# A head's attention laid anew on its five steps, in a fused attention, gated convolution and spatial-gating kernel

## The chip, the cores and the metric

The kernel runs on one core of one Trainium2 chip. The time is the device time of one execution, in microseconds (us). Five engines work at once, each through its own queue of instructions in order: TensorE (PE, matmuls), VectorE (DVE), ScalarE (ACT), GpSimd (POOL) and SyncE (SP, which issues the DMAs). They wait for one another through semaphores.

## The reference

Three layers in a row, all in float32, for a batch of 4, 576 tokens, 8 heads of 64.

```
cum    = cumsum(max(s, 0))                          # per head
scores = q k^T / 8 + min(-(cum_i - cum_j), 0), causal mask
attn   = softmax(scores);  x = attn v               # 32 heads -> x (4, 576, 512)

gate = sigmoid(causal conv of 5 taps over x)        # depthwise
x    = (gate * (x w_val)) w_out

h    = relu(x w_in);  u, v = halves of h            # 512 each
v    = (v - mean) / sqrt(var + 1e-6)
v_s  = w_spatial v + b_spatial                      # over tokens
out  = (u * v_s) w_out2
```

## The kernel before

**Data.** Every product is made of float32r parts: a value is split into a high part (a ScalarE copy) and a low part (VectorE or GpSimd subtracts), and TensorE multiplies the parts. `w_out` and `w_in` are first multiplied together (`comb_mm`, 8 tiles of 4 products each, evicted by `comb_evict`), as nothing lies between them.

**Steps.** All work is written out along one list of steps, in `run`. At each step every engine's queue gets its part of what is called, in the order of the calls. Nothing synchronizes the steps; they only set the order in each queue. A head takes five steps (`NT` = 5 tiles of query rows, the last of 64 rows; tile i has 128(i+1) keys, the last 576); 32 heads make 160 steps. A batch's mixer (everything after attention) takes 40 steps and lies beside the attention of the next batch; the last one runs alone.

**A head.** For tile i: `scores` (TensorE) fills a bank of `score`; VectorE reduces it to the negated row maximum (L851); ScalarE's `exp` (L725) reads the bank and writes `prob`; `turn` transposes `prob` on TensorE (L1000) into one of two banks of `turned`, from which ScalarE copies the high part `pt_hi` (L734) and VectorE then subtracts the low part `pt_lo` (L869). There are two score banks: tiles 0 and 2 use one, 1 and 3 the other, and tile 4 lies over both, so `scores` of a tile waits for the exp of the tile before it in its bank. The products with v (`pv_...`, L1009) add up in `attn_o`; ScalarE copies the lower half (L744) and VectorE adds the upper (L877). Beside that, the sums of the exps are inverted on VectorE (`invert_sums`), transposed (`turn_sums`, L1031), copied (`keep_sums`), stored to DRAM and loaded again spread over partitions (`store_sums`, `spread_sums`), and GpSimd multiplies two heads' x by them (L659).

Before the change the steps of a head g are: tile 0 scored in its step 0, 1 in 1, 2 and 3 in 2, 4 in 4. Its tiles are turned in the steps of the next head: 0 and 1 in step 0, then one a step. The products with v come in steps 3 and 4 of the next head and step 0 of the one after, the combination there too. In a step, TensorE's mixer products come first, then scores, then turns; ScalarE copies the turned tile and then makes the exp.

**The mixer.** `mixer_schedule` gives each operation its step, counted from the batch's end of attention. `lead` is called first in a step and `tail` last. The units of products are "val" (8), "v" (5, each in two halves), "u" (8), "spatial" (8, of 15 matmuls each) and "out" (8). A tap is one of the five VectorE operations of a channel block's convolution (L894, L897); `tanh` makes the gate of it. `x_hi` and `x_lo` split x. "val" and "spatial" units are evicted by VectorE (L914, L918), the others by ScalarE; `stats`, `norm` and `split` normalize and split v.

**Weights.** `weights` gives piece n its high part in step 2 + n on ScalarE and its low part a step later, on GpSimd for even n and VectorE for odd; SyncE loads a piece seven ahead. `COMB_STEPS` lists the steps of the combined products. The late pieces (`w_spatial`, `w_out2`) come from `LATE_FROM` on.

Of the kernel before, what the change touches and what calls it, by code (L numbers as in the profile page):

```python
# [30 lines left out]
TAPS = 5  # L31
# [56 lines left out]


def build(nc, q, k, v, s, w_val, conv_w, w_out_t, w_in, w_spatial, b_spatial, w_out2, out_t):  # L90
# [8 lines left out]
    NH = B * H  # L99
# [33 lines left out]
    TURNED_IN = [(0, 1), (2,), (3,), (4,), ()]  # L133
    SLOTS = NC + 2
    EARLY = 3

    ctx = ExitStack()
    with ctx:
# [269 lines left out]
        def run(do):  # L408
# [15 lines left out]
            def weights(step):  # L424
                for n in range(FIRST_LOADS, len(PIECES)):
                    at = WEIGHTS_FROM + n if n < LATE_PIECE else LATE_FROM + n - LATE_PIECE
# [12 lines left out]
            def early(step):  # L439
                g, i = divmod(step, NT)  # L440
                if g < NH and i == EARLY:
                    call("scores", g, i)
                    call("exp", g, i)

            def attention(step):
                g, i = divmod(step, NT)
                if i == 0 and 0 <= g - 2 < NH:
                    call("pv_rest", g - 2)
                if i == 2 and 0 <= g - 1 < NH:
                    call("turn_sums", g - 1)  # L450
                    call("keep_sums", g - 1)
                if g < NH and i != EARLY:
                    call("scores", g, i)
                if 0 <= g - 1 < NH:
                    for n in TURNED_IN[i]:
                        call("turn", g - 1, n)
                    if i == 3:
                        call("pv_first", g - 1)
                    if i == 4:
                        call("pv_second", g - 1)  # L460
                if g < NH and i != EARLY:
                    call("exp", g, i)
                if i == 0 and 0 <= g - 1 < NH:
                    call("invert_sums", g - 1)
                if i == 0 and 0 <= g - 2 < NH:
                    call("combine", g - 2)
                if i == 0 and g + 1 < NH:
                    call("scale_q", g + 1)
                if i == (0 if g == 0 else 1) and g + 1 < NH:
                    call("split_qk", g + 1)  # L470
                    call("place_qk", g + 1)
                if step == 0:
                    call("more_weights")
                if i == 2 and g + 2 < NH:
                    call("load_qk", g + 2)
                if i == 3 and 0 <= g - 1 < NH:
                    call("store_sums", g - 1)
                if i == 3 and g < NH:
                    call("split_v", g)
                    if g + 1 < NH:  # L480
                        call("load_v", g + 1)
                if i == 4 and 0 <= g - 1 < NH:
                    call("spread_sums", g - 1)
# [131 lines left out]
        def _(pool):  # L615
# [38 lines left out]
            def combine(g):  # L654
# [24 lines left out]
            run({"setup": setup, "weights_lo": weights_lo, "split_qk": split_qk, "split_v": split_v, "combine": combine,  # L679
# [4 lines left out]
        def _(act):  # L684
# [51 lines left out]
            def combine(g):  # L736
# [27 lines left out]
            def evict(b, alone, unit):  # L764
# [4 lines left out]
                if kind == "v":  # L769
# [3 lines left out]
                    elif b > 0:  # L773
# [15 lines left out]
            def split(b, alone, unit):  # L789
# [4 lines left out]
                else:  # L794
# [5 lines left out]
                 "exp": exp, "turn": turn, "keep_sums": keep_sums, "combine": combine, "x_hi": x_hi, "tanh": tanh, "evict": evict, "split": split,  # L800
# [143 lines left out]
        def _(pe):  # L944
# [76 lines left out]
            def pv_second(g):  # L1021
                pe.wait_ge(pt_lo_done, NT * (g + 1))
                pv_part(g, (0, 1), False, NT - 1)

            def pv_rest(g):
# [95 lines left out]
            def mm(b, alone, unit, half):  # L1121
# [6 lines left out]
                if half == 1 or unit[0] != "v":  # L1128
                    ins.then_inc(unit_done, 1)

            run({"setup": setup, "scores": scores, "turn": turn, "pv_first": pv_first, "pv_second": pv_second,
                 "pv_rest": pv_rest, "turn_sums": turn_sums, "comb_mm": comb_mm, "mm": mm})
# [32 lines left out]
```

## Time and profile before

| | us |
|---|---|
| median of 3 runs | 579.08 (578.79 to 579.66) |
| profiled execution | 577.76 |
| its span, first to last instruction | 576.0 |
| TensorE busy | 519.5 (90%) |
| VectorE busy | 369.8 (64%) |
| ScalarE busy | 330.2 (57%) |
| GpSimd busy | 263.2 (46%) |
| mean granted TensorE clock | 0.97 of full |

Busy shares are averages over stretches with different limits: the first batch's attention, which has only weight work beside it, three batches of attention with a mixer beside it, and the last mixer alone. They have to be read stretch by stretch. `turn_sums` occurs once a head, always in the same step of it (step 7, 12, 17, ... before the change), so that its starts cut the trace into heads.

### The profile page before, as it was taken

To read this page: it belongs to the slowest core of one execution; us is meant where nothing else is said; L and a number is where in the kernel's file an instruction comes from. 1 tells how busy PE (TensorE), PEld (TensorE's weight loads), DVE (VectorE), ACT (ScalarE), POOL (GpSimd) and SP (SyncE) were. 2 spreads that over 40 slices of the span, in tenths; PEclk is the share of its full clock that TensorE was granted. 3 is DMA by queue.
4 is the path that set the end of the run, shared out by engine and by line. 5 is a ranking of instruction groups with operands and counts; after the bars stand their busy time and mean duration, and the time that the engine had idled before them with its cause. 6 is when DMAs were issued, how large, how long until landed. Compare 5 with 4: busy or idle time off the path is not lost. (4 is left out here: it accounts for less than half of the span.)

```text
span 576.0 us, 10408 instructions
## 1 busy us (share of the span) xinstructions
PE 519.5 (90%) x3472; PEld 452.9 (79%) x3472; DVE 369.8 (64%) x726; ACT 330.2 (57%) x844; POOL 263.2 (46%) x247
## 2 busy tenths in 40 slices
PE   1758787878898899999999999999999999999998
PEld 1446565656886699998887899998877999997997
DVE  7346677776865866666758675768677757565240
ACT  4457666665584755676566656666666655523322
POOL 5244544433487664633556745445558544003100
PEclk9968999986998999999999999999999999999999
DMA  6753444432253333244333222343333320200002
GB/s 182 200 157 100 127 131 119 105 84 63 60 151 83 84 84 79 69 109 119 85 87 103 71 71 52 101 136 95 83 84 84 84 63 13 73 20 2 1 2 82
DMA packets 46887, 50.34 MB, mean 87 GB/s; under 512 B 24881, under 2 KB 29137, under 8 KB 46834
## 3 DMA queue, kind: packets, MB, share of 16 engines
q1 hardware_dynamic: 46834, 49.68, 32.2%
q8 instruction: 28, 0.46, 0.3%
q14 instruction: 25, 0.20, 0.1%
HBM read 25.83 MB, written 4.95 MB: 53 GB/s over the span
## 5 line engine op out<-in xcount | busy, mean ns | idle before, releaser
L725 ACT ACTIVATE prob<-score,neg_max 128x128 f32<-128x128 f32 (+4 forms) x159 | 90.2, 567 | 114.0 <-DVE neg_max L851 113.7
L869 DVE TENSOR_TENSOR pt_lo<-turned,pt_hi 128x128 fp32r<-128x128 f32 (+4 forms) x160 | 77.7, 489 | 69.7 <-ACT pt_hi L734 69.2
L851 DVE TENSOR_REDUCE neg_max<-score 128x1 f32<-128x128 f32 (+4 forms) x159 | 84.7, 533 | 40.0 <-PE score L981 35.1
L638 POOL TENSOR_TENSOR q<-raw,raw_hi 64x576 fp32r<-64x576 f32 x32 | 46.5, 1453 | 105.6 <-issue 60.7
L734 ACT ACTIVATE pt_hi<-turned 128x128 fp32r<-128x128 f32 (+4 forms) x160 | 66.8, 434 | 40.5 <-PE turned L1000 39.1
L979 PE MATMUL score<-k,q 68*128 68x256 f32 (+2 forms) x128 | 52.7, 412 | 30.8 <-ACT prob L725 17.2
L1000 PE MATMUL turned<-ident,prob 128*128 128x128 f32 (+1 forms) x480 | 71.1, 269 | 0.0
L1009 PE MATMUL attn_o<-pt_hi,v_hl 128*128 128x256 f32 (+2 forms) x224 | 66.9, 316 | 1.6 <-DVE pt_lo L869 1.6
L897 DVE SCALAR_TENSOR_TENSOR u_t<-x_t,taps,u_t 128x576 f32<-128x576 f32 x64 | 61.3, 957 | 0.7
L1041 PE MATMUL mix<-ws_hl,act_a 128*128 128x288 f32 (+1 forms) x405 | 59.2, 298 | 0.0
L1009 PE MATMUL attn_o<-pt_lo,v_hl 128*128 128x256 f32 (+2 forms) x224 | 59.1, 298 | 0.0
L406 POOL TENSOR_TENSOR act_b<-u_t,act_b 128x288 fp32r<-128x288 f32 x48 | 41.1, 861 | 37.9 <-ACT act_b L797 37.6
L979 PEld LDWEIGHTS score<-k,q 68*128 68x128 f32 x128 | 25.9, 202 | 38.4 <-issue 20.9
L659 POOL TENSOR_TENSOR x_t<-x_t,r_bc 128x576 f32<-128x576 f32 x16 | 25.7, 1605 | 66.2 <-DVE x_t L877 56.6
L1041 PEld LDWEIGHTS mix<-ws_hl,act_a 128*128 128x128 f32 (+1 forms) x405 | 55.0, 188 | 0.0
L1000 PEld LDWEIGHTS turned<-ident,prob 128*128 128x128 f32 (+1 forms) x480 | 48.3, 146 | 8.0 <-issue 6.0
L1041 PE MATMUL mix<-wc_hl,act_b 128*128 128x512 f32 (+1 forms) x204 | 54.4, 405 | 0.0
L1041 PE MATMUL mix<-act_b,wc_hl 128*128 128x288 f32 x312 | 46.2, 299 | 4.1 <-ACT work L776 4.1
L1041 PE MATMUL mix<-act_a,wv_hl 128*128 128x288 f32 x312 | 47.7, 303 | 1.0 <-DVE wc_hl L902 1.0
L1041 PE MATMUL mix<-act_b,w_hl 128*128 128x288 f32 x324 | 48.2, 298 | 0.0
L1009 PEld LDWEIGHTS attn_o<-pt_hi,v_hl 128*128 128x128 f32 x224 | 43.2, 193 | 6.0 <-DVE pt_lo L869 2.1
L651 POOL TENSOR_TENSOR v_hl<-v_raw,v_hl 128x320 fp32r<-128x320 f32 x32 | 37.0, 1155 | 23.8 <-ACT v_hl L716 23.6
(149 smaller groups left out, 1055.1 us busy)
## 6 DMA issues: line engine op xcount, KB each, us to landing
q<-raw_hi SPq DMA_DIRECT2D x64, 144.0 KB
k<-raw_hi SPq DMA_DIRECT2D x64, 144.0 KB
raw<-in_q SPq DMA_DIRECT2D x32, 144.0 KB, 2.8
raw<-in_k SPq DMA_DIRECT2D x32, 144.0 KB, 2.9
r_bc<-r_dram SPq DMA_DIRECT2D x32, 144.0 KB, 2.9
out<-work SPq DMA_DIRECT2D x32, 144.0 KB, 1.8
v_raw<-in_v SPq DMA_DIRECT2D x32, 128.0 KB, 2.1
u_t<-in_moe_w_in SPq DMA_DIRECT2D x7, 256.0 KB, 4.4
```

Source lines behind the costliest of these rows:

```text
L406: eng.tensor_tensor(lo, src, hi.bitcast(F32), ALU.subtract).then_inc(lo_done, 1)
L638: pool.tensor_tensor(q2[p][0:D, :], raw[0:D, :], raw_hi[0:D, :].bitcast(F32), ALU.subtract).then_inc(lo_made, 1)
L651: pool.tensor_tensor(v_hl[p][:, :, D:2 * D], v_raw[:, :, :], v_hl[p][:, :, 0:D].bitcast(F32), ALU.subtract).then_inc(v_lo_done, 1)
L725: act.activation(prob_view(i), score_view(g, i), ACT.Exp, bias=neg_max[p][0:rows[i], i:i + 1], accum_out=row_sum[p][0:rows[i], i:i + 1]).t ...
L734: act.activation(pt_view(pt_hi, i), turned_view((g + i) % 2, i), ACT.Copy).then_inc(pt_hi_done, 1)
L851: dve.tensor_reduce(neg_max[g % 2][0:rows[i], i:i + 1], score_view(g, i), AX_X, ALU.max, negate=True).then_inc(max_done, 1)
L869: dve.tensor_tensor(pt_view(pt_lo, i), turned_view((g + i) % 2, i), pt_view(pt_hi, i).bitcast(F32), ALU.subtract).then_inc(pt_lo_done, 1)
L897: dve.scalar_tensor_tensor(out=to, in0=src, scalar=w, in1=to, op0=ALU.mult, op1=ALU.add).then_inc(conv_step, 1)
L979: pe.matmul(score[:, base:base + n], q1[p][0:D + 4, qs], k1[p][0:D + 4, 0:n], start=True, stop=False)
L1000: ins = pe.transpose(turned[:, (g + i) % 2, j * rows[i]:(j + 1) * rows[i]], prob[0:rows[i], at:at + P], ident[0:rows[i], 0:rows[i]])
L1009: ins = pe.matmul(attn_o[:, O_OFF + lo:O_OFF + hi], v_hl[g % 2][:, j, :], t[:, at:at + hi - lo], start=(j == 0 and t is pt_hi), stop=(j == ...
L1041: ins = pe.matmul(o, a(ha), b(hb), start=(n == 0 and t == 0), stop=(n == len(pairs) - 1 and t == 2))
```

## The change

The five steps of a head are laid out anew (`scoring`, `turning`, `joining`, `moving` in place of `early` and `attention`):

- tiles 0 and 1 are scored in step 0, 2 in step 1, 3 in step 2, 4 in step 3, none in step 4;
- tiles are turned in the same head: 0 and 1 in step 2, 2 in step 3, 3 in step 4, and 4 in step 0 of the next head;
- `pv_first` stands in step 4, the rest of the products with v in step 1 of the next head (one call `pv` in place of `pv_second` and `pv_rest`), the combination in step 2, the multiplication by the inverted sums (now called `divide`) in step 3;
- in every step scores and exp come first on all engines, then turns, then the mixer's leading part; so ScalarE makes the exp before it copies a turned tile;
- splitting and placing q and k goes from step 1 of the head before to step 4, two heads before; loads and DMAs of the sums go with the new steps;
- the mixer starts two steps earlier, its taps, statistics, norms and splits get other steps, the combined products and late weight pieces too;
- `turn_sums` no longer waits for the combination; `pv_first` does.

```diff
-    for c, step in enumerate((1, 3, 4, 6)):
-        put(lead, step, "x_hi", c)
+    for c, step in enumerate((-1, 1, 2, 5)):
+        put(tail, step, "x_hi", c)
         put(tail, step, "x_lo", c)
-    for n, step in enumerate((-17, -16, -16, -14, -12, -11, -11, -9, -7, -6, -2, -2, -1, 1, 3) if first else
-                             (-22, -21, -21, -17, -16, -12, -11, -11, -9, -7, -2, -2, -1, 1, 3)):
-        put(tail, step, "tap", n // TAPS, n % TAPS)
-    for t, step in enumerate((7, 8, 8, 9, 9)):
+    for n in range(3 * TAPS):
+        put(tail, (-21 if first and n < TAPS else -16) + n, "tap", n // TAPS, n % TAPS)
+    for t, step in enumerate((5, 5, 6, 6, 7)):
         put(tail, step, "tap", 3, t)
-    for c, step in enumerate((-5, -4, 5, 10)):
+    for c, step in enumerate((-10, -5, 0, 8)):
         put(lead, step, "tanh", c)
-    step = 8
+    step = 6
...
-        put(tail, (18, 21, 22, 24, 26)[j], "stats", j)
-        put(tail, (21, 23, 24, 26, 28)[j], "norm", j)
-        put(tail, (23, 24, 25, 28, 29)[j], "split", ("v", j, 0))
+        put(tail, step + 2, "stats", j)
+        put(tail, step + 4, "norm", j)
+        put(tail, step + 5, "split", ("v", j, 0))
...
-    TURNED_IN = [(0, 1), (2,), (3,), (4,), ()]
+    SCORED_IN = [(0, 1), (2,), (3,), (4,), ()]
+    TURNED_IN = [(), (), (0, 1), (2,), (3,)]
...
-        COMB_STEPS = [6, 7, 9, 11] + [n for n in range(12, H * NT + 8) if n % NT != 0 and n != 17]
+        COMB_STEPS = [7, 9, 11, 12] + [n for n in range(13, H * NT + 6) if n % NT != 0 or n in (H * NT, H * NT + 5)]
-        LATE_FROM = H * NT + 8
+        LATE_FROM = H * NT + 7
+        LATE_STEPS = [LATE_FROM + n for n in (0, 1, 3, 5, 6, 8, 10, 11, 13)]
...
+            def scoring(step):
+                g, i = divmod(step, NT)
+                if g < NH:
+                    for n in SCORED_IN[i]:
+                        call("scores", g, n)
+                        call("exp", g, n)
+            def turning(step):
+                g, i = divmod(step, NT)
+                if i == 0 and 0 <= g - 1 < NH:
+                    call("turn_sums", g - 1)
+                    call("turn", g - 1, NT - 1)
+                    call("keep_sums", g - 1)
+                if g < NH:
+                    for n in TURNED_IN[i]:
+                        call("turn", g, n)
+            def joining(step):
+                g, i = divmod(step, NT)
+                f = g - 1
+                if i == 1 and 0 <= f < NH:
+                    call("pv", f)
+                    call("copy_low", f)
+                if i == 2 and 0 <= f < NH:
+                    call("combine", f)
+                if i == 3 and 0 <= f < NH:
+                    call("divide", f)
+                if i == 4 and g < NH:
+                    call("pv_first", g)
+                    call("invert_sums", g)
+            def moving(step):
+                g, i = divmod(step, NT)
+                f = g - 1
+                if step == 0:
+                    call("scale_q", 1)
+                    call("split_qk", 1)
+                    call("place_qk", 1)
+                    call("more_weights")
+                if step == 1:
+                    call("split_v", 0)
+                if i == 1 and 0 <= f < NH:
+                    call("store_sums", f)
+                if i == 1 and g + 2 < NH:
+                    call("load_qk", g + 2)
+                if i == 2 and g + 1 < NH:
+                    call("load_v", g + 1)
+                if i == 2 and 0 <= f < NH:
+                    call("spread_sums", f)
+                if i == 4 and g + 1 < NH:
+                    call("split_v", g + 1)
+                if i == 4 and g + 2 < NH:
+                    call("scale_q", g + 2)
+                    call("split_qk", g + 2)
+                    call("place_qk", g + 2)
...
+                scoring(step)
+                turning(step)
                 mixer(0, step)
                 comb(step)
-                attention(step)
-                early(step + 1)
+                joining(step)
+                moving(step)
                 weights(step)
-                if step == 7:
+                if step == 5:
                     call("bias_rows")
                 mixer(1, step)
...
-                pe.wait_ge(r_copied, g + 1)
+                wait(pe, r_copied, g)
+                wait(pe, o_added, g)
                 pe.wait_ge(pt_lo_done, NT * g + 2)
...
             def turn_sums(g):
                 pe.wait_ge(inv_done, g + 1)
-                wait(pe, o_added, g)
```

## Rows read from the trace of the kernel before

**Rows 1.** page, part 1: busy us of each engine, share of the span, instructions
```profile
PE 519.5 (90%) x3472; PEld 452.9 (79%) x3472; DVE 369.8 (64%) x726; ACT 330.2 (57%) x844; POOL 263.2 (46%) x247
```

**Rows 2.** windows: length, busy us (count) per engine, TensorE clock, DMA share, GB/s
```profile
24.37:46.85 22.48, 12.54 (x58) 9.22 (x56) 9.43 (x21) 10.64 (x26) 7.05 (x5) 0.75 0.46 121
...
46.85:137.26 90.41, 73.25 (x412) 54.70 (x411) 65.09 (x127) 58.50 (x151) 41.20 (x29) 0.92 0.42 109
...
46.85:142.64 95.79, 76.99 (x429) 57.51 (x427) 68.49 (x133) 62.73 (x161) 44.11 (x31) 0.91 0.41 107
...
221.53:342.28 120.75, 118.51 (x846) 105.68 (x844) 84.86 (x168) 76.53 (x202) 65.23 (x62) 1.00 0.34 90
...
326.14:342.28 16.14, 16.14 (x124) 15.09 (x122) 11.96 (x22) 10.37 (x28) 7.29 (x8) 1.00 0.30 75
...
373.39:387.55 14.16, 14.16 (x110) 13.12 (x108) 9.71 (x18) 9.44 (x24) 6.01 (x4) 1.00 0.49 138
```

**Rows 3.** timeline of PE: start us, us, engine, line, operation [idle before <- releaser]
```profile
35.50 0.76 PE L1041 MATMUL mix<-act_b,ws_hl 128*128 128x512 f32 x1 [4.16 <-DVE act_b L370]
...
44.29 0.47 PE L1041 MATMUL mix<-act_b,ws_hl 128*128 128x512 f32 x1 [3.35 <-DVE act_b L370]
...
142.64 1.65 PE L1041 MATMUL mix<-act_a,wv_hl 128*128 128x288 f32 x6
```

**Rows 4.** waits: us in total, times, longest us
```profile
PE score L979 <- ACT prob L725: 17.2, 19, 2.4
...
PE score L988 <- ACT prob L725: 6.0, 6, 1.7
...
PE mix L1041 <- DVE act_b L370: 7.5, 2, 4.2
...
DVE pt_lo L869 <- ACT pt_hi L734: 69.2, 99, 2.2
```

**Rows 5.** ScalarE's groups by form: count, busy us, mean ns, idle before
```profile
L725 ACT ACTIVATION_READ_ACCUMULATOR prob<-score,neg_max 128x1 f32 x128 | 25.5, 199 | 0.0
...
L725 ACT ACTIVATE prob<-score,neg_max 128x256 f32<-128x256 f32 x32 | 15.1, 471 | 15.3 <-DVE neg_max L851 15.1
...
L725 ACT ACTIVATE prob<-score,neg_max 128x512 f32<-128x512 f32 x32 | 22.0, 688 | 23.9 <-DVE neg_max L851 23.9
...
L725 ACT ACTIVATE prob<-score,neg_max 64x576 f32<-64x576 f32 x31 | 22.9, 737 | 67.2 <-DVE neg_max L851 67.2
...
L734 ACT ACTIVATE pt_hi<-turned 128x128 fp32r<-128x128 f32 x32 | 8.8, 275 | 25.1 <-PE turned L1000 25.1
...
L734 ACT ACTIVATE pt_hi<-turned 128x384 fp32r<-128x384 f32 x32 | 15.6, 488 | 8.8 <-PE turned L1000 8.5
...
L734 ACT ACTIVATE pt_hi<-turned 128x320 fp32r<-128x320 f32 x32 | 13.8, 431 | 1.4 <-PE turned L1000 1.4
```

**Rows 6.** page, part 5, VectorE's reduces and low parts, all forms together
```profile
L851 DVE TENSOR_REDUCE neg_max<-score 128x1 f32<-128x128 f32 (+4 forms) x159 | 84.7, 533 | 40.0 <-PE score L981 35.1
...
L869 DVE TENSOR_TENSOR pt_lo<-turned,pt_hi 128x128 fp32r<-128x128 f32 (+4 forms) x160 | 77.7, 489 | 69.7 <-ACT pt_hi L734 69.2
```

**Rows 7.** VectorE's groups by form
```profile
L897 DVE SCALAR_TENSOR_TENSOR u_t<-x_t,taps,u_t 128x576 f32<-128x576 f32 x64 | 61.3, 957 | 0.7
...
L877 DVE TENSOR_TENSOR x_t<-attn_o,x_t 64x576 f32<-64x576 f32 x32 | 24.0, 750 | 10.7 <-ACT x_t L744 10.6
...
L856 DVE TENSOR_SCALAR raw<-raw 64x576 f32<-64x576 f32 x32 | 15.1, 472 | 6.7 <-DMA raw<-in_k 6.2
...
L914 DVE SCALAR_TENSOR_TENSOR u_t<-u_t,mix 128x288 f32<-128x288 f32 x26 | 11.6, 444 | 5.6 <-PE mix L1041 5.6
```

**Rows 8.** line 897, the taps: duration ns min/median/max, first and last start
```profile
L897 DVE SCALAR_TENSOR_TENSOR u_t<-x_t,taps,u_t x64: 798/813/2025, 78.7 to 510.6; 128x576 f32<-128x576 f32 x64
```

**Rows 9.** timeline of VectorE, a tap and what follows it
```profile
101.26 0.81 DVE L897 SCALAR_TENSOR_TENSOR u_t<-x_t,taps,u_t 128x576 f32<-128x576 f32 x1
...
101.98 0.74 DVE L851 TENSOR_REDUCE neg_max<-score 64x1 f32<-64x576 f32 x1
```

More of the change, by code:

```diff
@@ L132, in build @@
     NS = len(SPLITS)
-    TURNED_IN = [(0, 1), (2,), (3,), (4,), ()]
+    SCORED_IN = [(0, 1), (2,), (3,), (4,), ()]
+    TURNED_IN = [(), (), (0, 1), (2,), (3,)]
     SLOTS = NC + 2
-    EARLY = 3
     ctx = ExitStack()
@@ L425, in weights @@
                 for n in range(FIRST_LOADS, len(PIECES)):
-                    at = WEIGHTS_FROM + n if n < LATE_PIECE else LATE_FROM + n - LATE_PIECE
+                    at = WEIGHTS_FROM + n if n < LATE_PIECE else LATE_STEPS[n - LATE_PIECE]
                     if step == at:
@@ L437, in comb @@
                         call("comb_evict", n)
-            def early(step):
+            def scoring(step):
                 g, i = divmod(step, NT)
[L441 to L445, printed above, removed]
+                if g < NH:
[3 more added lines that the diff above has]
+            def turning(step):
@@ L446, in attention @@
                 g, i = divmod(step, NT)
-                if i == 0 and 0 <= g - 2 < NH:
-                    call("pv_rest", g - 2)
-                if i == 2 and 0 <= g - 1 < NH:
+                if i == 0 and 0 <= g - 1 < NH:
                     call("turn_sums", g - 1)
+                    call("turn", g - 1, NT - 1)
                     call("keep_sums", g - 1)
-                if g < NH and i != EARLY:
-                    call("scores", g, i)
-                if 0 <= g - 1 < NH:
+                if g < NH:
@@ L455, in attention @@
                     for n in TURNED_IN[i]:
[L456 to L471, printed above, removed]
+                        call("turn", g, n)
[12 more added lines that the diff above has]
+                    call("invert_sums", g)
@@ L472, in attention @@
+            def moving(step):
+                g, i = divmod(step, NT)
+                f = g - 1
                 if step == 0:
+                    call("scale_q", 1)
+                    call("split_qk", 1)
+                    call("place_qk", 1)
                     call("more_weights")
-                if i == 2 and g + 2 < NH:
-                    call("load_qk", g + 2)
[L476 to L481, printed above, removed]
@@ L482, in attention @@
-                if i == 4 and 0 <= g - 1 < NH:
-                    call("spread_sums", g - 1)
+                if step == 1:
[3 more added lines that the diff above has]
+                if i == 1 and g + 2 < NH:
+                    call("load_qk", g + 2)
+                if i == 2 and g + 1 < NH:
+                    call("load_v", g + 1)
+                if i == 2 and 0 <= f < NH:
+                    call("spread_sums", f)
@@ L652, in split_v, with divide @@
                                    ALU.subtract).then_inc(v_lo_done, 1)
-            def combine(g):
+            def divide(g):
                 if g % 2 == 1:
@@ L677, in split @@
                     split_lo(pool, b, unit)
-            run({"setup": setup, "weights_lo": weights_lo, "split_qk": split_qk, "split_v": split_v, "combine": combine,
+            run({"setup": setup, "weights_lo": weights_lo, "split_qk": split_qk, "split_v": split_v, "divide": divide,
                  "stats": stats, "split": split})
@@ L734, in turn, with copy_low @@
                 act.activation(pt_view(pt_hi, i), turned_view((g + i) % 2, i), ACT.Copy).then_inc(pt_hi_done, 1)
-            def combine(g):
+            def copy_low(g):
                 a, h = divmod(g, H)
@@ L772, in evict @@
                         act.wait_ge(lo_done, NS * b + SPLIT[("val", n, 1)] + 1)
-                    elif b > 0:
+                    elif b == 0:
+                        wait_pieces(act, len(PIECES))
+                    else:
                         act.wait_ge(out_stored[2 * (n - NC + 1)], 16 * OUTS * b)
@@ L799, in _ @@
             run({"cumulate": cumulate, "bias_rows": bias_rows, "weights_hi": weights_hi, "split_qk": split_qk, "split_v": split_v,
-                 "exp": exp, "turn": turn, "keep_sums": keep_sums, "combine": combine, "x_hi": x_hi, "tanh": tanh, "evict": evict, "split": split,
+                 "exp": exp, "turn": turn, "keep_sums": keep_sums, "copy_low": copy_low, "x_hi": x_hi, "tanh": tanh, "evict": evict, "split": split,
                  "comb_evict": comb_evict})
@@ L1016, in pv_first, with pv @@
                 pe.wait_ge(v_lo_done, g + 1)
-                pe.wait_ge(r_copied, g + 1)
+                wait(pe, r_copied, g)
+                wait(pe, o_added, g)
                 pe.wait_ge(pt_lo_done, NT * g + 2)
                 pv_part(g, (0, 1), True, 1).then_inc(pv_first_done, 1)
-            def pv_second(g):
+            def pv(g):
                 pe.wait_ge(pt_lo_done, NT * (g + 1))
                 pv_part(g, (0, 1), False, NT - 1)
-            def pv_rest(g):
                 pv_part(g, (2, 3, 4), False, NT - 1).then_inc(pv_done, 1)
@@ L1129, in mm @@
                     ins.then_inc(unit_done, 1)
-            run({"setup": setup, "scores": scores, "turn": turn, "pv_first": pv_first, "pv_second": pv_second,
-                 "pv_rest": pv_rest, "turn_sums": turn_sums, "comb_mm": comb_mm, "mm": mm})
+            run({"setup": setup, "scores": scores, "turn": turn, "pv_first": pv_first, "pv": pv,
+                 "turn_sums": turn_sums, "comb_mm": comb_mm, "mm": mm})
 _INS = ["q", "k", "v", "s", "moe_w_val", "moe_conv_w", "moe_w_out", "moe2_w_in", "moe2_w_spatial",
```

## The prediction

> **What bounds the kernel now.** I read the shares of busy time first, then a table of stretches cut at the starts of `turn_sums`, then the waits, then single instructions. Over the span TensorE is busy 519.5 of 576.0 us [rows 1]. The stretches divide that [rows 2]. A whole overlapped batch, where attention and the mixer of the batch before run together, takes 120.75 us with TensorE busy 118.51 at full clock: TensorE sets the time there, and only 2.24 us a batch is idle. The first batch's attention is another regime. From 24.37 to 46.85 us TensorE is busy 12.54 of 22.48; over seven heads from 46.85 to 137.26 it is busy 73.25 of 90.41, VectorE 65.09. No engine is full there. The order in each queue sets the time. The waits say so [rows 4]: TensorE's scores wait for ScalarE's exp 17.2 + 6.0 us, and two combined-weight products wait 7.5 us for a weight's low part. Those two lie at 35.50 and 44.29 us [rows 3]. From where the mixer begins (142.64 us [rows 3]) the remaining work is TensorE's own, so the end is that work plus whatever TensorE loses; the change removes no matmul.
>
> **The change, part by part.** The sum is made for the profiled execution: 577.76 us, 1.8 more than its span. The median of the three runs is 1.3 above it; I move the median by the same difference.
>
> *(a) Combined-weight products on later steps.* They stood on steps 6, 7, 9, 11 and go to 7, 9, 11, 12; the pieces' own steps stay. The low part of piece 5 is made in step 8 and needed by the third product: one step later before, three after. Piece 7: made in step 10, needed in step 11 before, 12 after. The waits of 4.16 and 3.35 us [rows 3] hang on these two, and behind them in TensorE's queue stood a head's scores. They can go whole (-7.5), or come back as waits of the same scores for VectorE (0), because VectorE is busy only 9.43 of the 22.48 us but in long strings. I take -4.0. `bias_rows` moves from step 7 to 5 and may wait for its load there, beside a DMA wait that exists anyway: nothing.
>
> *(b) The mixer starts two steps earlier.* From step 12 to step 48 (46.85 to 142.64) is 35.6 steps in 95.79 us, 2.69 a step. Of that TensorE's attention work is small: a spatial head (15 matmuls a step) takes 16.14, one with 12 a step 14.16 [rows 2]; 15 matmuls more cost 1.98, 0.132 each, so 60 are 7.9 and a head's attention is 6.2, 1.25 a step. Two steps before the mixer less return 2 x (2.69 - 1.25) = -2.9. Between 0 (if the mixer then waits for its first input) and -2.9. In the new chain pv, combine, divide and x_hi lie on steps 1, 2, 3 and 5, x_lo on 5 and the product on 6; the DMA pair of the sums has steps 1 to 3. That fits, so I keep -2.9.
>
> *(c) Chain first: exp goes ahead of the turned tile's copy on ScalarE.* Before, ScalarE copied `pt_hi` and then made the exp, so VectorE's `pt_lo` followed its reduce nearly at once. After, in steps 0, 2 and 3 of a head VectorE's order is reduce, `pt_lo`, and `pt_lo` needs reduce, exp, `pt_hi` on ScalarE in turn. VectorE must be idle meanwhile, however much is queued behind (taps, evicts, combine). Durations from [rows 5], with 0.1 for the handovers: step 2: exp of tile 3 0.69 + read 0.10 beyond it + `pt_hi` 0.28 + 0.1 = 1.2, a little more for the second tile, 1.3; step 3: 0.74 + 0.10 + 0.49 + 0.1 = 1.4; step 0: exp 1 0.47 + 0.10 + `pt_hi` 0.43 + 0.1 = 1.1. That is 3.75 us of compulsory idle a head. Steps 1 and 4 have none. Before, the seven heads had 90.41 - 65.09 = 25.32 of VectorE idle, 3.62 each. So in the first batch the compulsory idle replaces an idle of the same size. Operations that follow one another start closer than they last (a tap at 101.26, the reduce at 101.98, for 0.81 [rows 9]), which takes perhaps 0.4 a head off; what is added is 0.5 for places where the queues still wait on each other. 3.84 against 3.62, times seven: +1.5. Bounds: -2.0 (no such places: 3.34) and +9 (each head also keeps the 1.2 or so by which the heads of before wait beyond one compulsory gap). What goes: tile 0's scores no longer stand one step behind tile 4's exp (tile 4 is now scored in step 3, step 4 scores nothing), which is most of the 23.2 us of score waits [rows 4]; late next is VectorE, not TensorE. `turn_sums` loses its wait for the combine; it is left waiting for `invert_sums`, queued on VectorE behind `pt_lo` 3. The wait for the combine passes to `pv_first`, two steps behind it, with the next head's scores queued after it: nothing.
>
> *(d) The same order in the overlapped batches.* Each has VectorE busy 84.86 of 120.75 [rows 2]; eight heads' compulsory idle add 30.0: 114.9, 95% of the time. On the mean it fits. It must also fit locally, as TensorE can only be led by about a step. A head costs VectorE five reduces 2.67, five `pt_lo` 2.44 [rows 6], combine 0.75 and scaling 0.47 [rows 7], 6.3, with the idle 10.1 (the two short ones of `invert_sums` I take as paid by the closer starts). A tap adds 0.72 (start to start [rows 9]), an evict of "val" or "spatial" 0.44 [rows 7]. Mixer steps 30 to 34 have five taps and five evicts now: 10.1 + 3.6 + 2.2 = 15.9 against TensorE's 16.14: just hidden. Steps 5 to 9 have the five taps of the last channel, one x_lo (as a combine, 0.75) and four evicts: 10.1 + 3.6 + 0.75 + 1.8 = 16.2 against 14.16: 2.0 not hidden. The other groups have 1 us or more to spare. Of the 2.24 idle before I leave half. So 2.0 + 1.1 - 2.24 = +0.9 a batch, and three such batches: +2.7. Bounds: -6.7 (all idle gone, the excess carried into the next head) and +15 (0.6 a head lost to coupling, near the 0.70 that one wait of `pt_lo` for `pt_hi` lasts: 69.2 over 99 [rows 4]).
>
> *(e) Moved and priced at nothing.* GpSimd's and SyncE's splits and placements of q and k go from step 1 of the head before to step 4 two heads before, so they have six steps instead of four; on SyncE they stand ahead of nothing but loads of two heads on. stats, norm and split of v come earlier, spread evenly; what consumes them keeps three steps. Late weight pieces are spread over 14 steps and are due at mixer step 30, as before. After the last attention TensorE is full before and after.
>
> The median tap lasts 0.81 and the mean 0.96, the longest 2.03 [rows 7, 8]; something blocks a few. The Trainium skill (SBUF — State Buffer, "SBUF: two separate sides") says that VectorE with two SBUF inputs and GpSimd share a port pair under an exclusive lock, so that the later of the two waits for the whole other instruction. That speaks against this change, since the splits of q and k now fall on step 4, and three taps of a batch fall there with them: by the rule VectorE would lose up to some 3 us a batch more, by the mean row 0.15 a tap, as today.
>
> Sum: -4.0 - 2.9 + 1.5 + 2.7 = -2.7. Profiled: 575.1; median: **576.4 us**.
>
> **The rivals.**
> *R1, slower: VectorE becomes the bound.* Place: `pt_lo` in steps 0, 2 and 3, waiting behind an exp that itself stands behind ScalarE's evicts and splits. If each of the three waits is 0.15 longer than its compulsory part, 0.45 a head over 31 heads is +14: 590.4. It decides early: from 0.13 a head (0.13 x 31 = 4) the kernel is slower than before. For it: the 95% of (d), and that VectorE already waits 69.2 us for `pt_hi` in the kind order. Against: TensorE's margin of about one step in most groups, and that the first batch's heads idle as much already. In the first batch the granted clock is 0.92 over the seven heads and 0.75 in the stretch before [rows 2], where TensorE idles most, and 1.00 in the overlapped batches. The Trainium skill (TensorE: Matmul & The Clock Gate, Part 1) says that an idle array falls to 1.2 GHz; so R1 would bring such stretches into the overlapped batches too, at a further price that no row here bounds.
>
> *R2, much faster: the queues never meet.* The weight waits go whole (-7.5), two steps -2.9, first batch -2.0, overlapped batches unchanged: -12.4, 566.7. For it: only 90.41 - 73.25 = 17 us of the seven heads is TensorE idle and nearly all of it waits for exp. Against: compulsory idle of VectorE stays.
>
> *R3, no change.* The ramp is bound by loads and by VectorE's own string, and the mixer's start is held by the sums' round trip through DRAM, so (a) and (b) bring nothing, while (c) and (d) cost nothing: 579.1. For it: 22.48 us for five steps, with DMAs in flight. Against: the step numbers of (a).
>
> **How the numbers follow.** Forecast 0.43, its own range 571 to 583; R1 0.25; R2 0.20; R3 0.12. About 0.2% (1.2 us) is what a measurement can tell from no change. Of the forecast's own case 0.6 lies under 577.9, 0.18 within the band, 0.22 above. Faster: 0.26 + 0.20 + 0.02 = 0.48; same: 0.08 + 0.07 = 0.15; slower: 0.09 + 0.25 + 0.03 = 0.37. The range takes in R2's value and most of R1's: 566 to 594.
>
> **What would show it.** (a): no TensorE wait for `act_b` low parts before the first head's combined tile is done, and `turn_sums` of head 1 before 43 us. (b): the first "val" product near 135 us. (c): `pt_lo` waits for `pt_hi` well above 69.2 us in total, near 32 x 3.75 = 120; score waits for exp far below 23; seven heads in 90 to 93 us. (d): overlapped batches of 120 to 122 us, with TensorE idle gathered in mixer steps 5 to 9. I am wrong if the overlapped batches grow by 3 us or more each or show a clock under 1.00 (R1), if the ramp keeps its 22 us (R3), or if batches fall under 119.

## The result, and the profile after

The changed kernel takes 628.81 us (628.38 to 630.34, 4 runs) against 578.93 of the kernel before on the same chip (578.61 to 579.66, 4 runs): 1.086 times as long (95% interval 1.084 to 1.089). 576.4 was forecast, with a range of 566 to 594.

Part 1 of the page, and the granted clock and busy slices of part 2, of the changed kernel:

```profile
PE 538.2 (86%) x3472; PEld 467.8 (75%) x3472; DVE 381.9 (61%) x726; ACT 323.0 (52%) x844; POOL 252.0 (40%) x247
...
PE   2586878767989889989799899978999999999998
...
PEclk9878888888789999999999999999999999999999
```

The matmuls are the same 3472. TensorE's busy time rose from 519.5 [rows 1] to 538.2 us, as more of them ran at the lower of its two clock levels (1.2 and 2.4 GHz): the mean granted clock fell from 0.97 to 0.945. The rest of the 50 us is idle. The windows are cut at the starts of the reciprocal in `invert_sums`, which occurs once a head. First come the first batch's heads 1 to 7 in the kernel before, cut in the same way, then the same heads and the second overlapped batch in the changed kernel.

```profile
41.94:118.71 76.77, 60.42 (x354) 44.60 (x355) 54.26 (x108) 50.34 (x131) 35.34 (x25) 0.97 0.43 115
```

```profile
42.29:136.94 94.65, 71.76 (x354) 55.63 (x354) 59.70 (x111) 49.38 (x131) 34.54 (x26) 0.82 0.36 97
292.75:427.40 134.65, 122.54 (x847) 107.74 (x845) 88.27 (x168) 74.50 (x202) 62.58 (x62) 0.99 0.31 81
```

Six heads of the first batch take 94.65 us where they took 76.77: 15.8 each against 12.8. TensorE's 354 matmuls in them last 71.76 us in place of 60.42, at a granted clock of 0.82 in place of 0.97, so part of the longer head is TensorE at its lower clock; no run took that part alone. VectorE's idle there is (94.65 - 59.70) / 6 = 5.8 us a head, against 3.75. An overlapped batch takes 134.65 where it took 120.75 [rows 2], with TensorE idle 12 us in it.

The waits of the whole kernel (us in total, times, longest):

```profile
DVE pt_lo L883 <- ACT pt_hi L746: 121.7, 105, 2.6
...
ACT raw_hi L723 <- DVE raw L870: 42.6, 24, 2.4
DVE neg_max L865 <- PE score L995: 31.5, 28, 4.2
PEld attn_o L1043 <- DVE row_inv L879: 30.8, 25, 2.1
PE attn_o L1043 <- DVE row_inv L879: 27.2, 23, 2.0
...
PE score L993 <- ACT prob L737: 22.4, 19, 7.2
...
PE score L1002 <- ACT prob L737: 13.7, 17, 2.0
```

L883, L746, L865, L1043, L723 and L870 are the lines 869, 734, 851, 1031, 711 and 856 of before. VectorE's wait for the high part went from 69.2 [rows 4] to 121.7, close to the 120 foretold. `turn_sums` (L1043) waited 2.4 us in all before, and for the combination; now it waits 27.2 for the inverse. The waits of scores for exp did not go; 23.2 became 36.1. ScalarE's wait to copy the scaled q (`raw_hi`) is new too; its row before was:

```profile
ACT raw_hi L711 <- DVE raw L856: 1.0, 2, 0.6
```

Before, VectorE scaled q in one step and ScalarE copied it in the next; now both are in step 4, with VectorE's part behind `invert_sums` and ScalarE's ahead of the next exp.

How these hang together shows in the chain of waits through one head of the first batch (start us, length, what the chain ran through; its pieces of "issue", time on no profiled work, are among those left out):

```profile
90.17 0.19 DVE row_inv L879
90.36 0.34 DVE raw L870
...
90.72 0.02 ACT raw_hi L723
...
91.31 0.15 ACT prob L737
...
91.81 0.69 PE score L993
...
92.95 1.39 PE mix L1053 x3
94.33 2.29 PE attn_o L1023 x10
96.63 0.59 PE score L993
...
97.74 0.70 DVE neg_max L865
...
99.05 0.19 ACT prob L737
99.24 0.44 ACT pt_hi L746 x2
...
100.20 0.69 DVE wc_hl L916
100.90 0.65 DVE x_t L891
101.55 0.68 DVE neg_max L865
...
103.08 0.38 ACT pt_hi L746
...
103.48 0.52 DVE pt_lo L883
...
104.57 0.75 DVE row_inv L877
```

The string runs: inverse, scaling of q, its copy on ScalarE, exp 0, scores 2, combined products, pv, scores 3, reduce 3, exp 3, copies, two other VectorE operations, reduce 4, exp 4, copy, low part, inverse. From one inverse to the next it passes through VectorE, ScalarE and TensorE in turn. (The view follows one chain back; it does not say how nearly another is as long.) VectorE's reduce at 97.74 had stood 4.20 us for scores that were queued behind pv, the rest of the products with v of the head before.

### The profile page after: what moved, and what is told of

Read it like the earlier page. It is cut to its first block, busy times and chain, and to the rows that moved or that the text cites. A ratio compares the mean times of both kernels' runs of the same rounds, so it can differ in the third digit from the quotient of the medians.

```text
span 626.6 us, 10373 instructions
## 1 busy us (share of the span) xinstructions
PE 538.2 (86%) x3472; PEld 467.8 (75%) x3472; DVE 381.9 (61%) x726; ACT 323.0 (52%) x844; POOL 252.0 (40%) x247
## 4 chain that ended last, share of the span: by engine, by line
PE 45%; DVE 27%; issue 11%; ACT 11%; DMA 3%; SPq 1%; POOL 1%; ACTq 0%; DVEq 0%; POOLq 0%
PE mix L1053 22%; PE attn_o L1023 7%; DVE neg_max L865 6%; DVE pt_lo L883 5%; PE attn_o L1053 4%; ACT pt_hi L746 4%; PE score L1053 3%; ACT prob L737 3%; DVE x_t L891 3%; DVE u_t L911 3%; PE score L993 3%; PE turned L1014 2%; PE score L994 2%; DVE act_a L895 2%; DVE row_inv L877 1%
## 5 line engine op out<-in xcount | busy, mean ns | idle before, releaser
L737 ACT ACTIVATE prob<-score,neg_max 128x128 f32<-128x128 f32 (+4 forms) x159 | 89.5, 564 | 157.6 <-DVE neg_max L865 157.1
L883 DVE TENSOR_TENSOR pt_lo<-turned,pt_hi 128x128 fp32r<-128x128 f32 (+4 forms) x160 | 77.6, 490 | 121.7 <-ACT pt_hi L746 121.7
L865 DVE TENSOR_REDUCE neg_max<-score 128x1 f32<-128x128 f32 (+4 forms) x159 | 82.3, 531 | 32.0 <-PE score L995 31.5
L993 PE MATMUL score<-k,q 68*128 68x256 f32 (+2 forms) x128 | 54.0, 422 | 34.5 <-ACT prob L737 22.4
L746 ACT ACTIVATE pt_hi<-turned 128x128 fp32r<-128x128 f32 (+4 forms) x160 | 64.0, 428 | 1.6 <-PE turned L1014 1.6
L1023 PE MATMUL attn_o<-pt_lo,v_hl 128*128 128x256 f32 (+2 forms) x224 | 64.6, 321 | 0.0
L911 DVE SCALAR_TENSOR_TENSOR u_t<-x_t,taps,u_t 128x576 f32<-128x576 f32 x64 | 64.3, 1004 | 0.4
L663 POOL TENSOR_TENSOR v_hl<-v_raw,v_hl 128x320 fp32r<-128x320 f32 x32 | 32.1, 1002 | 68.8 <-ACT v_hl L728 68.7
L1014 PEld LDWEIGHTS turned<-ident,prob 128*128 128x128 f32 (+1 forms) x480 | 50.2, 146 | 8.0 <-issue 1.9
L1053 PE MATMUL mix<-act_a,wv_hl 128*128 128x288 f32 x312 | 51.9, 319 | 3.4 <-DVE act_a L895 2.8
L1023 PEld LDWEIGHTS attn_o<-pt_hi,v_hl 128*128 128x128 f32 x224 | 48.7, 217 | 1.8 <-DVE pt_lo L883 0.4
L1023 PEld LDWEIGHTS attn_o<-pt_lo,v_hl 128*128 128x128 f32 x224 | 48.7, 217 | 1.6
```

The costliest lines, as they stand in the source:

```text
L663: pool.tensor_tensor(v_hl[p][:, :, D:2 * D], v_raw[:, :, :], v_hl[p][:, :, 0:D].bitcast(F32), ALU.subtract).then_inc(v_lo_done, 1)
L737: act.activation(prob_view(i), score_view(g, i), ACT.Exp, bias=neg_max[p][0:rows[i], i:i + 1], accum_out=row_sum[p][0:rows[i], i:i + 1]).t ...
L746: act.activation(pt_view(pt_hi, i), turned_view((g + i) % 2, i), ACT.Copy).then_inc(pt_hi_done, 1)
L865: dve.tensor_reduce(neg_max[g % 2][0:rows[i], i:i + 1], score_view(g, i), AX_X, ALU.max, negate=True).then_inc(max_done, 1)
L883: dve.tensor_tensor(pt_view(pt_lo, i), turned_view((g + i) % 2, i), pt_view(pt_hi, i).bitcast(F32), ALU.subtract).then_inc(pt_lo_done, 1)
L911: dve.scalar_tensor_tensor(out=to, in0=src, scalar=w, in1=to, op0=ALU.mult, op1=ALU.add).then_inc(conv_step, 1)
```

## The experiments

Each ratio is to the kernel before, measured together with the run (578.4 to 578.8 us). The changed kernel is 628.8.

**1. The sums turned at the end of step 0.**

```diff
                 if i == 0 and 0 <= g - 1 < NH:          # turning
-                    call("turn_sums", g - 1)
                     call("turn", g - 1, NT - 1)
-                    call("keep_sums", g - 1)
...
+                if i == 0 and 0 <= f < NH:              # joining
+                    call("turn_sums", f)
+                    call("keep_sums", f)
```

> One edit to the changed kernel: turn_sums and keep_sums are called at the end of a head's step 0 (behind the mixer's unit and the combined product) instead of ahead of the turn of tile 4. Theory T (TensorE's queue stands behind the inverted sums: 27.2 us of waits of L1043 for L879, with the turn of tile 4, the next product and the next scores queued behind it, and VectorE then idle for those scores): most of the 27 us and part of what follows comes back, 595 to 607 us, and those waits fall under 8 us. Theory C (VectorE's compulsory idle, exp ahead of the copy of the turned tile): the wait only moves, 624 to 630. Theory M (the mixer's new steps): 622 to 630.

619.5 us (1.071, 1.060 to 1.081). The waits of TensorE for the inverse fell from 27.2 to 7.0, but only 9 us came back. Part of that wait was slack that the next one took: the scores' wait for exp in the row of 22.4 grew to 39.4.

**2. The turned tile copied ahead of the exp.**

```diff
                 scoring(step)        # now scores alone
                 turning(step)
+                raising(step)        # exp of SCORED_IN
```

> One edit to the changed kernel: in each step ScalarE copies the turned tiles first and makes the exps after, as before the change; steps of a head stay. Theory C: VectorE's waits for pt_hi fall from 121.7 us to 70 or less, and since VectorE sets the pace in the first batch and about half of the overlapped ones, 590 to 603 us. Theory T: exp 4 is made later, so the sums are inverted no earlier, 620 to 632. Theory M: 620 to 630.

603.6 us (1.044, 1.036 to 1.051): 25.2 us of the 50 hang on this order alone. (`exp` is taken out of `scoring` and called in `raising`.) The waits of `pt_lo` fell from 121.7 to:

```profile
DVE pt_lo L889 <- ACT pt_hi L752: 42.2, 54, 2.0
```

Heads 1 to 7 gained little by it. There these waits fell from 21.5 us to 4.9, but VectorE's waits for scores rose from 12.6 to 20.9, and the window shrank only from 94.65 to:

```profile
41.88:134.36 92.48, 70.00 (x354) 54.48 (x354) 60.92 (x110) 50.73 (x131) 35.17 (x26) 0.83 0.37 99
```

**3. Mixer first in a step, as before the change.**

```diff
+                mixer(0, step)
+                comb(step)
                 scoring(step)
                 turning(step)
-                mixer(0, step)
-                comb(step)
```

> One edit to the changed kernel: in each step the mixer's leading part and the combined product are called ahead of scores, exps and turns again, on every engine. Under theory T and C alike this adds a unit of TensorE work between the inverse and turn_sums, and puts pv directly ahead of a product instead of ahead of tile 3's scores: T says 605 to 618 (the wait is covered by the unit, 1.6 to 2 us of it in the overlapped batches, nothing in the first batch beyond 0.7); C says 622 to 632 (ScalarE's order within the chain is the same); a theory that chain-first order itself is what costs says under 595.

641.1 us (1.108, 1.100 to 1.116). Slower than any of the three theories had it. Chain-first between engines' queues is not what costs; in this layout it is worth 12 us.

**4. The schedule of before for mixer, combined products and late pieces,** under the changed attention (`mixer_schedule`, `COMB_STEPS`, `LATE_FROM` restored).

> The changed kernel's attention with the schedule of before for the mixer, the combined products and the late weight pieces (the mixer starts at step 48 again). Theory M (taps, x_lo and statistics on wrong steps fill VectorE): under 605. Theories T and C: the loss is in the attention's own chain, 625 to 636, with a first batch as slow per head (15.4 to 15.8 us) as in the changed kernel.

634.7 us (1.097, 1.090 to 1.105). So the loss is in the attention, and that group of edits returns 6 us there.

**5. Edits 1 and 2 together.**

> The two edits of the first two runs together: turned tiles copied ahead of the exps, turn_sums and keep_sums at the end of step 0. If the two losses are separate (25.2 and 9.3 us of the changed kernel's 628.8), 594 to 597. If the wait for the sums was only a wait that the late pt_lo caused, nothing beyond the first edit: 602 to 605. If the chain of a head in the first batch is bound elsewhere (pv ahead of tile 3's scores), its heads stay at 14.5 to 15 us in both cases.

594.5 us (1.029, 1.021 to 1.036): 34.3 us back against 25.2 + 9.3. They are separate losses. The six heads of the first batch took 89.78 us, 15.0 each.

**6. And pv behind tile 3's scores.**

```diff
-                if i == 1 and 0 <= f < NH:
+                if i == 2 and 0 <= f < NH:
                     call("pv", f)
                     call("copy_low", f)
-                if i == 2 and 0 <= f < NH:
+                if i == 3 and 0 <= f < NH:
                     call("combine", f)
-                if i == 3 and 0 <= f < NH:
+                if i == 4 and 0 <= f < NH:
                     call("divide", f)
```

> As the run before, and pv and the copy of its lower half in step 2 of the next head (behind tile 3's scores and the first turns), combine in step 3, divide in step 4. Theory S (a head of the first batch is one serial chain, and the ten matmuls of pv, 2.3 us at the lower clock, stand in it ahead of tile 3's scores while VectorE waits 4.2 us for these): first batch heads fall by 1.5 to 2.5 us to about 12.5 to 13, 580 to 590. Rival: VectorE or ScalarE is full, and the heads fall by under 0.5 us: 593 to 598.

584.1 us (1.009, 1.005 to 1.014), 10.5 less than the run before. Heads 1 to 7 took 80.37 us, 9.4 less; that is nearly all of it.

**7. v loaded and split a step earlier** (steps 1 and 3 in place of 2 and 4), on the changed kernel.

> The changed kernel with v loaded in step 1 and split in step 3 instead of 2 and 4. In the changed kernel invert_sums' first operation (a 128x5 add, 0.16 us alone) has a mean of 0.36 us and ends within 0.05 us of the end of a GpSimd operation in most heads, the split of v in the first batch. If it is held by GpSimd and stands in the head's chain, its mean falls under 0.25 and the kernel to 618 to 625. If only the order of records is so, 626 to 631.

639.5 us (1.107, 1.101 to 1.113). A miss: 10.6 us slower. The mean of the add in `invert_sums`, 0.36 us before the edit, only fell to 0.34, and TensorE's waits for the inverse rose to 43.4. The edit puts the copy of v on ScalarE into step 3, between exp 4 and the copy of tile 3; it does not tell of GpSimd's hold alone.

**8. Edit 6 alone, on the changed kernel.**

> The changed kernel with pv and copy_low in step 2, combine in step 3, divide in step 4, nothing else. Theory S: first batch heads 13 to 14 us instead of 15.4, overlapped batches unchanged, 612 to 620. Rival (VectorE's compulsory idle alone sets the first batch): 626 to 631.

609.4 us (1.054, 1.048 to 1.059): 19.4 us, more than expected. Six heads of the first batch took 89.5 us in place of 94.65, 5 us of it; the rest came in the overlapped batches, where I had expected none.

**9. v split in step 0 of its own head,** on the changed kernel.

```diff
-                if i == 4 and g + 1 < NH:
-                    call("split_v", g + 1)
+                if i == 0 and 0 < g < NH:
+                    call("split_v", g)
```

> The changed kernel with v split in step 0 of its own head instead of step 4 of the head before; its load stays. GpSimd's split of v then no longer runs beside invert_sums in the first batch. If GpSimd holds VectorE's 128x5 add there, its mean falls from 0.36 us to under 0.30 and the first batch gains some 0.5 us a head: 621 to 627. If the split only followed the same chain, 627 to 632 and the mean stays.

623.6 us (1.077, 1.071 to 1.083), and the add's mean 0.30: 5 us. This edit too moves ScalarE's copy of v together with GpSimd's part, so the 5 us are not shown to be the hold's alone.

**10. The order of edit 2 put into the kernel before:** `exp` called right behind `scores`, ahead of the turned copies, nothing else.

```diff
                 if g < NH and i != EARLY:
                     call("scores", g, i)
+                    call("exp", g, i)
...
-                if g < NH and i != EARLY:
-                    call("exp", g, i)
```

> The kernel before with one edit: in each step exp is called ahead of the turn of the other head's tile, so ScalarE makes it before it copies the turned tile. Theory C (exp ahead of the copy makes VectorE wait for ScalarE wherever the two share a step): VectorE's waits for pt_hi rise from 69 to over 100 us; three of five steps of a head have both, and since the overlapped batches had VectorE 70% busy, part shows: 585 to 600. Rival (the cost of 25 us in the changed kernel was that of its single chain per head, and two heads interleaved hide it): 577 to 583.

626.4 us (1.082, 1.077 to 1.087). It slows the kernel before by 48 us, nearly as much as the whole change does, and far more than either reading had it. Its waits:

```profile
ACT prob L724 <- DVE neg_max L850: 184.4, 128, 6.2
DVE pt_lo L868 <- ACT pt_hi L733: 135.3, 125, 2.7
```

and one step of it on ScalarE, then on VectorE:

```profile
94.51 0.58 ACT L724 ACTIVATE prob<-score,neg_max 128x384 f32<-128x384 f32 x1 [1.07 <-DVE neg_max L850]
94.98 0.19 ACT L724 ACTIVATION_READ_ACCUMULATOR prob<-score,neg_max 128x1 f32 x1
95.08 0.59 ACT L733 ACTIVATE pt_hi<-turned 128x512 fp32r<-128x512 f32 x1
```

```profile
95.70 0.69 DVE L868 TENSOR_TENSOR pt_lo<-turned,pt_hi 128x512 fp32r<-128x512 f32 x1 [1.23 <-ACT pt_hi L733]
96.31 0.68 DVE L850 TENSOR_REDUCE neg_max<-score 128x1 f32<-128x512 f32 x1
```

The turned tile was ready before 93.2. ScalarE waits 1.07 for the reduce, VectorE then 1.23 for exp and copy: they take turns. With the copy first, ScalarE copies while VectorE reduces.

**11. Chain-first order in the kernel before,** copy still ahead of exp: scores, turns and exps ahead of the mixer's leading part, products with v behind.

> The kernel before with its scores, turns and exps (copy still ahead of exp) called ahead of the mixer's leading part and the combined product in every step, products with v and the rest behind them; steps unchanged. If chain-first order is itself good (it was worth 12 us in the changed layout), it is worth 2 to 8 us here: 571 to 577. If it was good there only because one head's chain set the pace, 577 to 581, or worse.

588.6 us (1.018, 1.014 to 1.022), 10 us slower. The 12 us of run 3 belong to the new layout. VectorE's combine now waited for ScalarE's lower copy 32.8 us in all, against 10.6 before. That copy waits for the products with v, which now stand behind scores, turns and the mixer's product.

**12. All three edits and number 9.**

> The third stack (turned tiles copied ahead of exps, turn_sums late, pv in step 2) with v split in step 0 of its own head. If GpSimd's hold of invert_sums matters once the rest of the chain is short, 578 to 583; if turn_sums, now late, leaves room for the inverse, 583 to 586 with no gain.

579.5 us (1.003, 1.000 to 1.005): level with the kernel before.

**13. `invert_sums` at the head of step 4,** alone on the changed kernel; **14.** the same on the stack of 12.

> The changed kernel with invert_sums at the head of step 4 instead of behind pt_lo of tile 3, the mixer's evict and pv_first's place. If turn_sums' wait is a matter of its place in VectorE's queue, it does the work of the first experiment (9.3 us): 616 to 621, and the 27 us of waits fall under 12. If exp 4 itself is late, 625 to 630.

> The last stack (copy ahead of exp, turn_sums late, pv in step 2, v split in step 0) with invert_sums at the head of step 4, ahead of the stretch in which GpSimd's divide holds it. If that hold delays what is queued behind it on VectorE (pt_lo, taps), 574 to 578; if there is slack, 578.5 to 581.

Alone 621.0 us (1.073, 1.071 to 1.075), with TensorE's waits for the inverse down to 12.5. On the stack 575.9 us, 0.994 (0.992 to 0.997) of the kernel before. The new layout, freed of these orders, is slightly ahead of the kernel before; how much of that is term (a), run 15 tells.

**15. Term (a) alone:** the kernel before with the combined products on 7, 9, 11, 12 and on.

```diff
-        COMB_STEPS = [6, 7, 9, 11] + [n for n in range(12, H * NT + 8) if n % NT != 0 and n != 17]
+        COMB_STEPS = [7, 9, 11, 12] + [n for n in range(13, H * NT + 8) if n % NT != 0]
```

> The kernel before with the combined products on steps 7, 9, 11, 12 and on, nothing else: term a of the prediction alone. If it is real: the two waits of 4.16 and 3.35 us go, 573 to 577. If the ramp is bound by the engines' strings and the loads, 577.5 to 580.

573.4 us, 0.991 (0.987 to 0.994): 5.3 us faster than the kernel before and the fastest of all. The stack of run 14 has these steps too and stands at 575.9, so beyond (a) the new layout is not shown to gain anything. Of the two waits, 7.5 us [rows 4], this is left:

```profile
PE mix L1041 <- DVE act_b L370: 2.0, 1, 2.0
```

**16. The mixer's new spacing alone:** the kernel before with the changed `mixer_schedule`, every step two later.

> The kernel before with the changed kernel's mixer schedule, all of it two steps later so that it starts at step 48 as before: taps one a step, statistics and splits of v early. In the changed layout the schedule of before cost 6 us more. If the spacing is good by itself: 573 to 577. If only the two steps were: 577.5 to 581. If even spacing puts taps beside spatial evicts and costs: over 581.

588.9 us (1.018, 1.015 to 1.021), 10 us slower. An overlapped batch takes 125.77 where it took 120.75:

```profile
265.99:391.76 125.77, 120.27 (x847) 107.06 (x846) 83.82 (x168) 76.94 (x203) 65.51 (x61) 0.99 0.34 87
```

The longest wait of TensorE in it, 2.7 us, is for the low part of x (L880) ahead of the mixer's first product; x_lo had been put one step, not two, ahead of that product. The rest of the 10 us stays open. The changed kernel has x_lo one step ahead too. What of run 4's 6 us belongs to the earlier start was not tried apart.

## Why the prediction was wrong

**The bound.** That TensorE sets the overlapped batches and the queues' order the first one was read rightly. That the end is TensorE's work plus what it loses also held: the matmuls did not change.

**(a), -4.0.** Right, alone: -5.3 in the kernel before. Under the longer head the ramp gained nothing that lasted (head 1's reciprocal at 42.29 us, at 41.94 before). The sign named for it, `turn_sums` of head 1 before 43 us, came true (42.54), but says little, as `turn_sums` has step 10 there now and had 12.

**(b), -2.9.** Not shown. The first "val" product came at 159.79 us, not near 135, for the heads ahead of it were longer. Before it came at 141.21; the row at 142.64 [rows 3], from which the term was worked out, is a later part of the same product, which changes the term by 0.1.

**(c), +1.5 for seven heads: a step that failed.** Measured: +17.9 for six (76.77 to 94.65). The compulsory idle was sized rightly: 3.75 us a head was put down, and in heads 1 to 7 the waits of `pt_lo` for `pt_hi` are 21.5 us, 3.6 each. What failed is that it "replaces an idle of the same size", with 0.5 us a head for "places where the queues still wait on each other". VectorE's idle came to 5.8 a head, so those places took 2.2: VectorE's wait for scores behind pv is 12.6 us in those six heads. TensorE's wait for the inverse (10.2 us) and ScalarE's for the scaled q (10.0 us) lie on the same string of waits. And the compulsory idle was not what set the time there: with it mostly gone (run 2) the heads gained 2.2 us in all, and the wait for the scores behind pv grew. Only with pv moved behind them as well did they gain another 9.4 (run 6). In the kernel before, the same idle put in by exp first did cost, 12.4 us in these heads (run 10). I had also written that `turn_sums` "is left waiting for `invert_sums`, queued on VectorE behind `pt_lo` 3", and gave this no price. It costs 8 to 9 us in the whole kernel (runs 1 and 13).

**(d), +2.7 for three batches: the larger failure.** The table has the time from the reciprocal of head 1 to that of head 7, and from head 8 to head 31, which is the three overlapped batches but for their last head.

| us | heads 1 to 7 | heads 8 to 31 |
|---|---|---|
| before | 76.8 | 356.6 |
| changed | 94.7 | 387.4 |
| copy first (run 2) | 92.5 | 366.6 |
| copy first, sums late (run 5) | 89.8 | 360.4 |
| and pv later (run 6) | 80.4 | 360.7 |
| pv later alone (run 8) | 89.5 | 374.3 |
| before, exp first (run 10) | 89.1 | 386.7 |

The overlapped part lost 30.8 us, 8 to 14 a batch, and 20.8 of it come back with the copy ahead of the exp. So here the compulsory idle did cost. Its size was right again: VectorE's waits for `pt_hi` in one batch are 31.1 us against the 30.0 put down, and were 17.0 before. The sentence that failed is "On the mean it fits". Busy time and these waits make 88.27 + 31.1 = 119.4 us, 99% of the old 120.75; the 95% of the forecast took the old busy time, 84.86. Even so the batch took 134.65, so VectorE idled another 15 and TensorE 12. My reading, which no run takes apart, is that a queue that must stop at fixed places cannot lend that time to its neighbours, and that TensorE can be led too little to cover it.

**(e)** The moved splits of q and k were priced at nothing, and VectorE's scaling and ScalarE's copy, which go with them, were not looked at. ScalarE's wait for the scaled q went from 1.0 to 42.6 us and lies on the string of the first batch. What it costs stays open: no run moved it alone, and with the other orders undone it is still 51.5 us (run 14). The split of v had no price of its own; in step 0 of its own head it returns 5 us.

**The rivals.** R1 named the place and the mechanism: `pt_lo` in steps 0, 2 and 3. Its price, three waits longer by 0.15 us each, 0.45 a head, had no row behind it and left out what is queued behind the waits; 50 us over 31 heads are 1.6. Its sign, batches that grow by 3 us or more, came true. Its reasons "against" were the same error as in (c). R2 and R3 fell. By the runs, of the 50 us: exp ahead of the copy 25, pv ahead of tile 3's scores 10 to 19 (on and off the other edits), the place of `turn_sums` and `invert_sums` 8 to 9, the split of v 5. These lean on one another and need not add up. Undone together they leave 575.9, so nothing large is open.

## What to carry to other kernels

Where two engines hand work back and forth, put first on each the operation whose input is already there. ScalarE can copy a tile turned long ago while VectorE reduces; behind the exp, the same copy made both engines take turns, for 25 us in one layout and 48 in the other. Before idle time is set off against idle time, follow one unit of work all the way round and price every wait on it; taking one away may only lengthen the next, as in heads 1 to 7 of run 2. And an engine whose work and compulsory stops come to 95% of the time should not be counted as fitting: here the batch grew by 14 us.

## What the hardware showed that was not expected

A GpSimd operation held up a tiny VectorE one. `invert_sums`' add over 128x5 values takes 0.16 us alone; in the changed kernel its mean was 0.36. On the timeline:

```profile
58.22 0.85 POOL L663 TENSOR_TENSOR v_hl<-v_raw,v_hl 128x320 fp32r<-128x320 f32 x1
58.38 0.72 DVE L877 TENSOR_SCALAR row_inv<-row_sum 128x5 f32<-128x5 f32 x1
59.13 0.19 DVE L879 RECIPROCAL row_inv<-row_inv 128x5 f32<-128x5 f32 x1
```

GpSimd ends at 59.07, the add at 59.10. In 19 of 32 heads the add ends within 0.05 us of the end of a GpSimd operation that had started before it, and in the kernel before in none. The Trainium skill (SBUF — State Buffer, "SBUF: two separate sides") has it that GpSimd shares a pair of ports with a VectorE operation that is in a 2-port mode or has two SBUF inputs, and that whichever of the two starts first keeps them for the whole instruction. These 19 heads agree, if the add, which has one tensor as input, runs in such a mode; that no run here shows. In three heads a GpSimd operation over 128x1 values ran across the whole add, which still took 0.16 to 0.18 us, so not every GpSimd operation held it. In the prediction I weighed that rule for the taps alone. They lost 3.0 us in all (61.3 [rows 7] to 64.3), while the add stood on the head's own chain.

TensorE's clock followed the idling: granted 0.82 over heads 1 to 7, against 0.97 before, and in the overlapped batch 0.99 against 1.00 [rows 2].
